# Six MoE chunks written out in a row in place of an engine loop with conditional arms

## Chip, cores and metric

The kernel runs on one core of one Trainium2 chip. The metric is the device time of one launch in microseconds (us), as the median of several runs.

## What is computed

Three stages follow each other. Sliding-window attention (4 batches, 8 heads, 576 positions, head size 64, window 64) gives x, one row of 512 for each of 2304 tokens. A dense gated layer maps it to new rows, and a mixture of 8 experts, one chosen per token, gives the output.

```
x = attention(q, k, v)                       # [2304, 512]
a = x @ w1 ; b = x @ w2                      # [2304, 1024]
x = (a * b @ w3) @ w_out                     # [2304, 512]
logits = x @ w_gate ; e = argmax(logits)     # 8 experts
h  = max(x @ w1[e], 0)
out = gate_w * sigmoid(x @ w_output_gate)[e] * (h @ w2[e])
```

## The kernel before

Every fp32 product is made of three TensorE matmuls (`product3`, L428 to L431): the high part of one factor by the high part of the other, and the two mixed products of a high and a low part. ScalarE (ACT) rounds a tile to its high part on the way out of PSUM, VectorE (DVE) subtracts to get the low part. TensorE (PE) is given its work by an order written out by hand, and the other engines follow by semaphores.

The program has these stages.

1. The fold: w3 and w_out are multiplied into one matrix W (`Wh`, `Wl`), together with the gate columns. Beside it runs the attention of batch 0.
2. The chunks. The 2304 rows of the dense layer are six chunks of 384 (`CH`). Two batches of 576 rows make one pass of three chunks (`NSUP` = 2 passes, `NCH` = 3 chunks in each). For each chunk `chunk` runs 8 hidden tiles of 24 matmuls (x by w1 and x by w2, `hidden_tile`), then 6 row tiles of 24 matmuls (a*b by W, `row_tile`), 14 steps in all. The first chunk of a pass, and the third chunk of the first pass, also carry the attention of one batch, one piece per step (`attend` before the step's own work: scores, L479; `attend_end` behind it: transposes, L489, and the product with v, L500). The second chunk of a pass and the last chunk of all carry none. The last chunk (`final`) also prepares the weights of expert 0 and, in `rank` (L557), begins the routing.
3. Routing: DVE computes each token's place in a list sorted by expert (L953 to L1034), with two small groups of matmuls (L560, L571, and L630 later).
4. The slot loop (`for_slots`, L299): one turn per 128 sorted tokens, with a gather of rows, two expert products (`hidden`, `project`) and a scatter. SyncE (SP) loads the weights of the next expert into `raw` (L413).

PE, ACT, DVE and GpSimd (POOL) each run the chunks through `for_chunks` (L238 to L245). In the kernel before, this is a loop of the engine itself: its body holds the code of chunk 0, of chunk 1, and two arms under a condition, one for the third chunk of the first pass, and one for the third chunk of the second pass (which is `final`). Four chunks of code therefore stand in each engine's program, and six are run. The number of the pass, `si`, is a register, so a chunk's waits compare a semaphore with a value that is computed from it.

At the start of each chunk PE waits for the last low part of the attention (`o_lo`), for the row tiles of the chunk before to be copied out of PSUM (`xB_ok`, `xA_ok`) and for the weights (`w12_lo`). The first chunk of a pass wants every ACT copy of the chunk before (`xA_ok` at `cc * CT + 1`), since its first hidden tile writes the banks that those copies read; the other chunks want all but the last two (L514). The copies are L730.

SP has its own loops for loading q, k, v and the expert weights.

Of the kernel before, what the change touches and what calls it, by code (L numbers as in the profile page):

```python
# [29 lines left out]
def build(nc, B, H, S, qT_in, kT_in, v_in, w1, w2, w3T_in, w_out, w_outT, w_gate, w_ogate, ew1, ew2, out):  # L30
# [13 lines left out]
    NSUP = N // SUPER  # L44
    CH = 384
    NCH = SUPER // CH
# [23 lines left out]
    with ctx:  # L70
# [164 lines left out]

        def for_chunks(eng, chunk):  # L238
            with eng.Fori(0, NSUP) as si:
                chunk(si * NCH, 0, si * 2 + 1, si * 2 + 1, 1, False)  # L240
                chunk(si * NCH + 1, 1, si * 2 + 2, None, 0, False)
                with eng.If(si < NSUP - 1):
                    chunk(si * NCH + 2, 2, si * 2 + 2, si * 2 + 2, 0, False)
                with eng.If(si > NSUP - 2):
                    chunk(si * NCH + 2, 2, si * 2 + 2, None, 0, True)  # L245


        def group_cols(k, parity):
# [69 lines left out]
        def _(sp):  # L318
# [5 lines left out]
            def load_w12(i):  # L324
                _, _, wr, src, kt = w12[i]
                if i >= KD:
                    sp.wait_ge(wo_lo, KF)
                sp.dma_start(wr[:, kt * FF:(kt + 1) * FF], src[kt * P:(kt + 1) * P, :]).then_inc(w12_in[i], 16)
# [96 lines left out]
        def _(pe):  # L425
# [131 lines left out]
            def rank():  # L557
# [2 lines left out]
                pe.matmul(bank[4][:, 0:TE], upper[:, :], oh[:, :], start=True, stop=True)  # L560
                pe.matmul(bank[5][:, 0:TE], ones[:, :], oh[:, :], start=True, stop=True).then_inc(rt_pe, 1)

            for_chunks(pe, chunk)

            pe.wait_ge(xA_ok, NT + 1)

# [73 lines left out]
        def _(act):  # L640
# [28 lines left out]
            def hi_w12(i):  # L669
                wh, wl, wr, _, kt = w12[i]  # L670
                ws = slice(kt * FF, (kt + 1) * FF)
                act.wait_ge(w12_in[i], 16)
                act.activation(wh[:, ws], wr[:, ws], ACT.Copy).then_inc(w12_hi, 1)
# [45 lines left out]
            def chunk(cc, c, batches, b, parity, final):  # L719
# [18 lines left out]
                for n, tt, i in row_tiles:  # L738
                    around(attend, attend_end, b, KF + i, parity, lambda: row_tile(i, n, tt))

            for_chunks(act, chunk)


            act.wait_ge(rt, 2)
# [62 lines left out]
        def _(dve):  # L807
# [36 lines left out]
            def lo_w12(i):  # L844
                wh, wl, wr, _, kt = w12[i]
                ws = slice(kt * FF, (kt + 1) * FF)
                dve.wait_ge(w12_hi, i + 1)
                dve.tensor_tensor(wl[:, ws], wr[:, ws], f32(wh[:, ws]), ALU.subtract).then_inc(w12_lo, 1)
# [56 lines left out]
            def chunk(cc, c, batches, b, parity, final):  # L905
# [22 lines left out]
                for n, tt, i in row_tiles:  # L928
                    around(attend, attend_end, b, KF + i, parity, lambda: row_tile(i, n, tt))

            for_chunks(dve, chunk)


            step = [0]
# [153 lines left out]
        def _(pool):  # L1088
# [49 lines left out]
            def attend(b, k, parity):  # L1138
                if k < NG:
                    pool.wait_ge(rec_ok, b * NG + (k + 1))  # L1140
                    pv = prob[k % 4][:, :].rearrange("p (i c) -> p i c", c=P)
                    pool.tensor_tensor(pv, pv, rec[:, k % 4 * 3:k % 4 * 3 + 3].unsqueeze(2).broadcast_to([P, 3, P]), ALU.mult).then_inc(p_ok, 1)  # L1142


            def split_lo(e, part):
                for c in range(NP1):
                    lo, hi = wcol(e, part, 1, c * PC), wcol(e, part, 0, c * PC)
                    pool.wait_ge(ew_hi[part], e * NP1 + c + 1)
                    pool.tensor_tensor(wbuf[:, lo:lo + PC], raw[part * NP1 + c][:, :], f32(wbuf[:, hi:hi + PC]),
                                       ALU.subtract).then_inc(ew_lo[part], 1)  # L1150
# [4 lines left out]
            def chunk(cc, c, batches, b, parity, final):  # L1155
                if b is not None:
                    for k in range(NG):
                        attend(b, k, parity)
                if final:
                    split_lo(0, 1)  # L1160
                for t in range(CT):
                    pool.wait_ge(xA_ok, cc * CT + (t + 2))
                    pool.wait_ge(xB_ok, cc * CT + (t + 2))
                    pool.dma_start(x_dram[bass.ds(cc * CH + t * P, P), :], x_sb[t][:, :]).then_inc(x_stored[t], 16)
                for t in range(CT):
                    pool.wait_ge(x_stored[t], cc * 16 + 16)
                pool.sem_inc(x_free, 1)

            for_chunks(pool, chunk)


            pool.wait_ge(idx_ok, 1)
# [82 lines left out]
```

## Time and profile before

| | |
|---|---|
| median of 3 runs | 778.92 us |
| the 3 runs | 777.67, 778.92, 780.96 us |
| span of the profiled execution, first to last instruction | 779.9 us |
| TensorE busy in the span | 731.2 us |
| mean granted TensorE clock | 0.970 |
| instructions in the profile | 15017 |

No time of the profiled execution other than its span is given; the span stands 1.0 us above the median of the runs. Times in a profile are from the start of the span. A busy time of PE counts overlapping matmuls once; a matmul starts before the end of the one ahead of it, so the distance between two starts is what one costs. "issue" as the releaser of an idle time says that the engine waited for nothing that the profile shows.

### The profile page before, as it was taken

Reading aid. Unit: us, or ns where it says so; the run is one execution under the profiler, and the core shown is the slowest. Engines: PE = TensorE matmul, PEld = TensorE weight load, DVE = VectorE, ACT = ScalarE, POOL = GpSimd, SP = SyncE. Lnnn points to the kernel's source line nnn. Section 1 sums busy time; section 2 is a strip of 40 time slices with the busy share of each in tenths; the row PEclk is TensorE's granted clock in tenths of the full one; section 3 lists DMA queues with packets and bytes.
Section 4 is the critical chain, followed back from the end, with each engine's and each line's share of the span. In section 5 each row is a group of like instructions: output and inputs, shape, how many; then the busy total and the mean of one; then the engine's idle time right before and its main releaser. Section 6 shows DMA issues by size and latency. Waiting matters only on the chain.

```text
span 779.9 us, 15017 instructions
## 1 busy us (share of the span) xinstructions
PE 731.2 (94%) x4832; PEld 670.9 (86%) x4833; DVE 333.0 (43%) x633; ACT 298.1 (38%) x720; POOL 141.3 (18%) x199
## 2 busy tenths in 40 slices
PE   6999999999999959999998975799999999999994
PEld 5999999999999959999998975688888888888883
DVE  3577444322154414541211279454456654562120
ACT  3577444422144414442201242044354554542221
POOL 7022011100111101111000054312221222121111
PEclk9999999999999979999999996699999999999998
DMA  9986222310112421206001052244446572611110
GB/s 292 234 245 168 57 61 77 95 41 1 42 32 58 114 76 32 58 28 224 34 7 38 0 194 104 94 149 151 147 136 217 200 234 88 219 32 40 30 41 27
DMA packets 64204, 80.27 MB, mean 103 GB/s; under 512 B 23501, under 2 KB 43981, under 8 KB 64144
## 3 DMA queue, kind: packets, MB, share of 16 engines
q1 hardware_dynamic: 59104, 64.01, 26.9%
q0 software_dynamic: 5040, 15.47, 5.9%
q8 instruction: 37, 0.61, 0.4%
q14 instruction: 23, 0.19, 0.1%
HBM read 70.03 MB, written 10.49 MB: 103 GB/s over the span
## 4 chain that ended last, share of the span: by engine, by line
PE 92%; DVE 4%; issue 2%; ACT 1%; DMA 0%; POOL 0%; DVEq 0%; POOLq 0%; ACTq 0%
PE bank L429 26%; PE bank L431 25%; PE bank L430 25%; PE bank L479 5%; PE bank L500 3%; PE bank L599 2%; PE bank L489 2%; DVE scll L1013 1%; PE bank L579 1%; PE bank L441 1%; PE bank L630 1%; PE bank L571 0%; DMA w3r<-in_w3T 0%; PE bank L467 0%; PE bank L463 0%
## 5 line engine op out<-in xcount | busy, mean ns | idle before, releaser
L429 PE MATMUL bank<-Wh,abh 128*128 128x272 f32 (+1 forms) x288 | 84.3, 293 | 0.0
L651 ACT ACTIVATE prob<-prob,nmx 128x128 f32<-128x128 f32 x144 | 56.3, 392 | 71.8 <-DVE nmx L821 71.8
L431 PE MATMUL bank<-Wh,abl 128*128 128x272 f32 (+1 forms) x288 | 82.4, 286 | 0.0
L430 PE MATMUL bank<-Wl,abh 128*128 128x272 f32 (+1 forms) x288 | 82.1, 285 | 0.0
L1142 POOL TENSOR_TENSOR prob<-prob,rec 128x384 f32<-128x384 f32 x48 | 39.8, 830 | 227.2 <-DVE rec L831 227.2
L429 PE MATMUL bank<-wbuf,xsTh 128*128 (+1 forms) x176 | 71.6, 407 | 0.7 <-DVE xsTl L1040 0.7
L1050 DVE TENSOR_TENSOR hTl<-bank,hTh 128x512 fp32r<-128x512 f32 x44 | 28.4, 686 | 101.2 <-ACT hTh L764 97.5
L902 DVE TENSOR_TENSOR wbuf<-raw,wbuf 128x1024 f32 (+1 forms) x56 | 66.0, 1222 | 12.8 <-ACT wbuf L716 12.8
L911 DVE TENSOR_TENSOR ab_f<-bank,a_sb 128x384 f32<-128x384 f32 x48 | 26.8, 558 | 104.2 <-PE bank L431 104.2
L429 PE MATMUL bank<-wbuf,hTh 128*128 x176 | 70.7, 402 | 0.0
L429 PE MATMUL bank<-xTh,w1h 128*128 128x384 f32 x192 | 67.8, 353 | 2.1 <-issue 2.0
L431 PE MATMUL bank<-wbuf,xsTl 128*128 (+1 forms) x176 | 69.7, 396 | 0.0
L430 PE MATMUL bank<-wbuf,xsTh 128*128 (+1 forms) x176 | 69.2, 393 | 0.0
L431 PE MATMUL bank<-wbuf,hTl 128*128 x176 | 68.9, 391 | 0.0
L430 PE MATMUL bank<-wbuf,hTh 128*128 x176 | 68.7, 390 | 0.0
L430 PE MATMUL bank<-xTl,w1h 128*128 128x384 f32 x192 | 65.5, 341 | 0.0
L431 PE MATMUL bank<-xTh,w1l 128*128 128x384 f32 x192 | 65.3, 340 | 0.0
L429 PE MATMUL bank<-xTh,w2h 128*128 128x384 f32 x192 | 64.3, 335 | 0.0
L430 PE MATMUL bank<-xTl,w2h 128*128 128x384 f32 x192 | 64.3, 335 | 0.0
L431 PE MATMUL bank<-xTh,w2l 128*128 128x384 f32 x192 | 64.2, 335 | 0.0
L716 ACT ACTIVATE wbuf<-raw 128x1024 f32 (+1 forms) x64 | 63.7, 1054 | 0.0
L724 ACT ACTIVATE abh<-ab_f 128x384 fp32r<-128x384 f32 x48 | 25.2, 525 | 90.1 <-DVE ab_f L911 90.1
(181 smaller groups left out, 1582.7 us busy)
## 6 DMA issues: line engine op xcount, KB each, us to landing
raw<-in_expert_w SPq DMA_DIRECT2D x64, 512.0 KB, 4.4
qbd<-in_qT SPq DMA_DIRECT2D x32, 144.0 KB, 3.7
kT<-in_kT SPq DMA_DIRECT2D x16, 288.0 KB, 4.1
x_rows<-x_sb POOLq DMA_DIRECT2D x18, 256.0 KB, 2.7
w3r<-in_w3T SPq DMA_DIRECT2D x8, 512.0 KB, 3.6
vA<-in_v SPq DMA_DIRECT2D x16, 256.0 KB, 3.0
vB<-in_v SPq DMA_DIRECT2D x16, 256.0 KB, 3.5
wo<-in_w_out SPq DMA_DIRECT2D x8, 256.0 KB, 6.9
```

The lines of the kernel that those rows point to most:

```text
L429: pe.matmul(dst, lh, rh, start=first, stop=False)
L430: pe.matmul(dst, lh, rl, start=False, stop=False)
L431: return pe.matmul(dst, ll, rh, start=False, stop=last)
L479: mm = pe.matmul(bank[4][:, (i % 3) * P:(i % 3 + 1) * P], qbd[r][:, i * P:(i + 1) * P], kT[r][:, key_start(i):key_start(i) + P], start=Tru ...
L500: mm = pe.matmul(bank[6 + k % 2][h * D:(h + 1) * D, i * WIN:(i + 1) * WIN], vt[:, h * D:(h + 1) * D], pT[(k - 1) % 2][:, i * P + h * WIN:i ...
L651: ex_i = act.activation(prob[k % 4][:, cols], prob[k % 4][:, cols], ACT.Exp, bias=nmx[:, row], accum_out=sums[:, row])
L716: act.activation(wbuf[:, bass.ds(wcol(e, part, 0, c * PC), PC)], raw[part * NP1 + c][:, :], ACT.Copy).then_inc(ew_hi[part], 1)
L724: act.activation(abh[:, f * CH:(f + 1) * CH], ab_f[f % 2][:, :], ACT.Copy).then_inc(ab_hi, 1)
L902: dve.tensor_tensor(wbuf[:, bass.ds(wcol(e, part, 1, c * PC), PC)], raw[part * NP1 + c][:, :], f32(wbuf[:, bass.ds(wcol(e, part, 0, c * PC ...
L911: dve.tensor_tensor(ab_f[f % 2][:, :], hidden_bank(c, f, 1)[:, 0:CH], a_sb[f % 2][:, :], ALU.mult).then_inc(ab_ok, 1)
L1050: dve.tensor_tensor(hTl[last][:, cols], bank[3 + n][:, :], f32(hTh[last][:, cols]), ALU.subtract).then_inc(hT_lo, 1)
L1142: pool.tensor_tensor(pv, pv, rec[:, k % 4 * 3:k % 4 * 3 + 3].unsqueeze(2).broadcast_to([P, 3, P]), ALU.mult).then_inc(p_ok, 1)
```

## The change

`for_chunks` no longer takes an engine and no longer opens a loop. It calls `chunk` six times in Python, with numbers in place of the register, so that each engine's program holds the six chunks one behind the other. The order of work is the same, and so are all waits; the values waited for are now constants. SP's loops and the slot loop stay as they are. The file is one line shorter, so that line numbers behind L245 are one less (L479 of before is L478 now).

```diff
-        def for_chunks(eng, chunk):
-            with eng.Fori(0, NSUP) as si:
-                chunk(si * NCH, 0, si * 2 + 1, si * 2 + 1, 1, False)
-                chunk(si * NCH + 1, 1, si * 2 + 2, None, 0, False)
-                with eng.If(si < NSUP - 1):
-                    chunk(si * NCH + 2, 2, si * 2 + 2, si * 2 + 2, 0, False)
-                with eng.If(si > NSUP - 2):
-                    chunk(si * NCH + 2, 2, si * 2 + 2, None, 0, True)
+        def for_chunks(chunk):
+            for cc in range(NSUP * NCH):
+                si, c = divmod(cc, NCH)
+                final = cc == NSUP * NCH - 1
+                batches = si * 2 + (1 if c == 0 else 2)
+                b = None if c == 1 or final else batches
+                chunk(cc, c, batches, b, 1 if c == 0 else 0, final)
...
-            for_chunks(pe, chunk)
+            for_chunks(chunk)
...
-            for_chunks(act, chunk)
+            for_chunks(chunk)
...
-            for_chunks(dve, chunk)
+            for_chunks(chunk)
...
-            for_chunks(pool, chunk)
+            for_chunks(chunk)
```

Two places of PE's program show what moves. The first is the end of a pass. (Names ending in h and l are high and low parts; `L239` is the loop, `L242` and `L244` are the two conditions.) Before, behind the code of chunk 2 (the first arm) PE leaves the arm and, in the first pass, jumps from the row `L244 COMPARE_AND_BRANCH` over the second arm, 351 rows of the program:

```order
L430 MATMUL bank<-Wl,abh 128x256
L431 MATMUL bank<-Wh,abl 128x256
L242 UNCONDITIONAL_BRANCH
L244 COMPARE_AND_BRANCH
L513 ISA [waits o_lo]
L514 REGISTER_ALU [waits xB_ok]
L429 MATMUL bank<-xTh,w1h 128x384 [waits W_lo,w12_lo,xA_ok]
```

It lands on the row `L239 REGISTER_ALU`, and the branch behind that takes it back to the loop's start, some 1615 rows up:

```order
L430 MATMUL bank<-Wl,abh 128x256
L431 MATMUL bank<-Wh,abl 128x256
L244 UNCONDITIONAL_BRANCH
L239 REGISTER_ALU
L239 COMPARE_AND_BRANCH
```

```order
L239 ISA
L513 ISA [waits o_lo]
L476 ISA [waits w12_lo,xA_ok,xB_ok]
L477 REGISTER_ALU [waits qk_in0]
L479 MATMUL bank<-kT_68,qbd_66 128x128 [waits masked]
```

Now, on PE, from the last row tile of chunk 2 to chunk 3:

```order
L428 MATMUL bank<-Wh,abh 128x256
L429 MATMUL bank<-Wl,abh 128x256
L430 MATMUL bank<-Wh,abl 128x256
L478 MATMUL bank<-kT_68,qbd_66 128x128 [waits w12_lo,qk_in0,xA_ok,masked,xB_ok,o_lo]
L478 MATMUL bank<-kT_68,qbd_66 128x128 x2
L428 MATMUL bank<-xTh,w1h 128x384 [waits W_lo]
```

The branches and register instructions are gone, and the scores of the next batch stand right behind the last matmul of chunk 2, with the same waits.

The second place is PE between chunk 4 and chunk 5. Before, the first condition is false in the second pass, so PE jumps from its row over the whole first arm, 457 rows, to the row `L244 COMPARE_AND_BRANCH` shown above and goes on into chunk 5 from there:

```order
L429 MATMUL bank<-Wh,abh 128x256
L430 MATMUL bank<-Wl,abh 128x256
L431 MATMUL bank<-Wh,abl 128x256
L242 COMPARE_AND_BRANCH
L513 ISA [waits o_lo]
L514 REGISTER_ALU [waits xB_ok]
```

Now the matmul that opens chunk 5 follows chunk 4 directly:

```order
L429 MATMUL bank<-Wl,abh 128x256
L430 MATMUL bank<-Wh,abl 128x256
L428 MATMUL bank<-xTh,w1h 128x384 [waits w12_lo,xA_ok,W_lo,xB_ok,o_lo]
L429 MATMUL bank<-xTl,w1h 128x384
L430 MATMUL bank<-xTh,w1l 128x384
```

PE's program grows from 2444 rows to 3120.

## Rows read from the trace of the kernel before

**Rows 1.** The page: PE's busy time, its clock by fortieths, the chain's shares.

```profile
PE 731.2 (94%) x4832; PEld 670.9 (86%) x4833; DVE 333.0 (43%) x633; ACT 298.1 (38%) x720; POOL 141.3 (18%) x199
...
PEclk9999999999999979999999996699999999999998
...
PE 92%; DVE 4%; issue 2%; ACT 1%; DMA 0%; POOL 0%; DVEq 0%; POOLq 0%; ACTq 0%
```

**Rows 2.** The waits: three of PE's (total us, times, longest).

```profile
PE bank L479 <- issue: 8.3, 1, 8.3
...
PE bank L560 <- DVE oh L961: 5.2, 1, 5.2
...
PE bank L429 <- issue: 2.0, 1, 2.0
```

**Rows 3.** The timeline, 275 to 290 us (start, duration, engine; idle before).

```profile
275.35 0.49 ACT L659 ACTIVATE pT<-bank 128x384 f32<-128x384 f32 x1
...
275.89 0.20 PEld L500 LDWEIGHTS bank<-pT,vB 128*64 128x64 f32 x4 [0.22 <-ACT pT L659]
...
279.21 0.28 PE L431 MATMUL bank<-Wh,abl 128*128 128x256 f32 x1
...
279.53 0.38 ACT L730 ACTIVATE x_sb<-bank 128x256 f32<-128x256 f32 x1 [2.69 <-PE bank L431]
...
287.84 1.64 PE L479 MATMUL bank<-kT,qbd 128*128 128x128 f32 x6 [8.35 <-issue]
...
289.60 0.52 PE L430 MATMUL bank<-xTl,w1h 128*128 128x384 f32 x1
```

**Rows 4.** The timeline of PE, 412 to 416 us.

```profile
412.19 0.28 PE L430 MATMUL bank<-Wl,abh 128*128 128x256 f32 x1
412.31 0.28 PE L431 MATMUL bank<-Wh,abl 128*128 128x256 f32 x1
...
414.57 0.41 PE L429 MATMUL bank<-xTh,w1h 128*128 128x384 f32 x1 [1.98 <-issue]
...
415.41 0.52 PE L430 MATMUL bank<-xTl,w1h 128*128 128x384 f32 x1
```

**Rows 5.** Windows cut from chunk starts to ACT copies: us, engines, PEclk, DMA, GB/s.

```profile
157.17:202.61 45.44, 45.44 (x293) 45.44 (x292) 10.45 (x22) 8.54 (x17) 0.54 (x1) 1.00 0.04 11
361.59:407.04 45.45, 45.45 (x293) 45.45 (x292) 10.45 (x22) 8.54 (x17) 0.54 (x1) 1.00 0.24 90
414.57:461.66 47.09, 46.97 (x288) 46.78 (x288) 17.18 (x29) 15.74 (x24) 6.02 (x3) 0.96 0.17 56
85.85:152.86 67.01, 67.01 (x541) 64.43 (x540) 31.13 (x81) 30.34 (x112) 10.74 (x13) 1.00 0.23 65
208.01:275.02 67.01, 67.01 (x541) 64.42 (x540) 30.79 (x80) 30.32 (x111) 11.08 (x14) 1.00 0.24 69
287.84:357.28 69.44, 69.33 (x539) 66.23 (x540) 30.78 (x80) 30.07 (x110) 10.54 (x13) 0.97 0.13 38
```

**Rows 6.** The DMA queues that bring instructions: 279.5 to 288, then 412.4 to 414.6.

```profile
q8 instruction: 3, 0.05, 3.5%
q14 instruction: 5, 0.04, 1.8%
...
q14 instruction: 1, 0.01, 1.5%
```

**Rows 7.** All DMA queues in 530 to 740 us, and the slot loop's scatters there.

```profile
q1 hardware_dynamic: 8320, 20.97, 30.5%
q0 software_dynamic: 2720, 7.88, 11.3%
...
out<-y_sb,sidc POOLq DMA_INDIRECT x17, 2.8
```

**Rows 8.** A short idle time of PE, and the window that holds it.

```profile
506.21 0.49 PE L429 MATMUL bank<-wbuf,xsTh 128*128 x1 [0.66 <-DVE xsTl L1040]
...
504.00:508.00 4.00, 3.34 (x21) 2.69 (x20) 1.66 (x4) 0.98 (x2) 1.21 (x2) 1.00 0.16 50
```

## The prediction

> **What bounds the kernel now.** I read the page first. TensorE is busy for 731.2 of 779.9 us and holds 92% of the chain that ended last [rows 1]. So the time is TensorE's, and a change counts only for what it takes out of, or puts into, TensorE's own row of work. The interesting part of the chain's shares is small: "issue" 2%, time in which an engine waited for nothing that the profile shows. The clock line has one dip between the start and the routing stage, a 7 in the fifteenth fortieth, which is 273 to 292 us.
>
> Next the list of waits, for PE alone. In the stretch of the chunks (86 to 475 us) it has two entries under "issue": 8.3 us once before the scores L479, and 2.0 us once before L429. The other long one there, 5.2 us before L560, is for DVE's routing work [rows 2]. The edit touches no operation of that work.
>
> Then the timeline at those two entries. The first is the end of the first pass: the last matmul of chunk 2 starts at 279.21 and the first scores of chunk 3 at 287.84 [rows 3]. The second lies between chunk 4 and chunk 5: 412.31 to 414.57 [rows 4]. Both are places where PE's program jumps, over an arm of 351 rows and back over 1615 rows at the first, over an arm of 457 rows at the second. Last I cut windows that hold equal work at each pass, and asked which DMA queues move in the gaps. The first shows what a gap costs behind it, the second what the engines are waiting for.
>
> **What the change removes.**
>
> *The jump back, directly.* PE cannot start chunk 3 right behind chunk 2, with or without the loop: its first hidden tile writes the banks that the last ACT copy reads, and it waits for that copy. The copy L730 runs from 279.53 to 279.91 [rows 3]. How long PE needs from ACT's end to its own start I take from the same rows: pT ends at 275.35 + 0.49 = 275.84 and L500 that waits for it starts at 275.89, so 0.05. Chunk 3 can start at 279.91 + 0.05 = 279.96. It starts at 287.84. Removed: **7.88 us**. All other conditions of that start are older: no wait but this one is listed there, and the profile calls the time issue. In the gap eight packets go over the instruction queues [rows 6]: the engines are fetching the code that they jumped to.
>
> *The jump back, behind it.* After the gap the clock is at its lower level (1.2 of 2.4 GHz): a matmul of 384 columns shows 0.52 us at 289.60. What that costs is read off equal work. From the first scores of a chunk with attention to its second L730, chunk 0 takes 67.01 us and chunk 2 67.01, both at clock 1.00; chunk 3 takes 69.44 at 0.97 [rows 5]. Removed, if TensorE does not idle long enough for the clock to fall: 69.44 - 67.01 = **2.43 us**. This holds a short second pause in it too.
>
> *The jump over the arm, directly.* Between chunk 4 and chunk 5 nothing has to be waited for (the copies that chunk 5 wants are two older ones). The distance between starts of row matmuls is 412.31 - 412.19 = 0.12, so chunk 5 could start at 412.43; it starts at 414.57 [rows 4]. Removed: **2.14 us**. One instruction packet falls into the gap [rows 6].
>
> *The jump over the arm, behind it.* The clock falls again (0.52 us for a matmul at 415.41, [rows 4]). From chunk start to first L730 chunk 1 takes 45.44 us and chunk 4 45.45, chunk 5 takes 47.09 at clock 0.96 [rows 5]. The last chunk is the one with `rank`, but that comes behind the fourth row tile, whose result this first L730 copies, so the TensorE work is equal. Removed: 47.09 - 45.45 = **1.64 us**.
>
> *Register work.* All engines lose the additions and register compares of the waits. On PE they cost nothing now: chunks 0, 1, 2 and 4 are busy for all of their windows (45.44 of 45.44, 67.01 of 67.01) [rows 5]. On ACT, DVE and POOL they stand in idle time, since these engines are busy for at most half of any such window. I set 0.
>
> **What it adds.** Two more chunks of code are fetched in place of being jumped back to. The first pass runs its code straight through and PE never idles in the windows of chunks 0 to 2 [rows 5], so fetching in a line is covered by the matmuls at hand. Chunk 4 is run straight through as well, while the expert weights come in (90 GB/s against 11 in chunk 1), and takes 45.45 against 45.44, so that load does not uncover it. If that cover failed once at a place, it would cost what the small gap costs, 2.14 + 1.64 = 3.8 us; not less than 0, since nothing here can speed a full row of matmuls up.
>
> What stays is the true wait at chunk 3: TensorE's last start 279.21 plus 0.12 to 279.96, some 0.6 us. Does it lower the clock? The nearest row is an idle time of 0.66 us at 505.5, and the window around it is at clock 1.00 [rows 8], while 1.98 us at 414.57 is followed by the lower level. I take no loss; the bound is one fall, 1.64 to 2.43 us.
>
> The chunk stage feeds later ones by semaphores alone. Routing and slot loop start from the end of the last chunk's tiles, and all of it moves forward as a block. The q, k and v loads of batch 3 are issued from the progress of batch 2 and have no row in PE's waits; they lose 8 us of slack at chunk 3, but at chunk 2, which starts with no gap in front of it, loads issued in the same rhythm leave PE busy for all 67.01 us. The eight loads of expert 0's weights follow the last attention tile, which also moves, and are wanted only at the end of the last chunk.
>
> **Sum.** 7.88 + 2.43 + 2.14 + 1.64 = 14.09 us. The span would go from 779.9 to 765.8; the median of the runs stands 1.0 below the span of before, so I predict 778.92 - 14.09 = **764.8 us**, 1.8% less.
>
> **The rivals.**
>
> 1. *One part of the gain is not got* (chance 0.12). Either the 0.6 us wait at chunk 3 does lower the clock, or one fetch in the straight code comes late, in one place where loads are heavy. Speaking for it: chunks 3 and 5 have never run directly behind their predecessors, and rows 8 is a single case, in the slot stage. Against: no idle time in the straight windows. Times: 764.8 + 2.4 = 767.2, or 764.8 + 3.8 = 768.6.
>
> 2. *The gaps are not due to the jumps* (0.03), but to some condition that the profile does not see at the start of chunks 3 and 5; then it stays and the time is 778.9. For it: "issue" is only what is left when no releaser is found. Against: the instruction packets in the gaps, the absence of any gap at chunks 1, 2 and 4, which check the same semaphores, and that the two gaps stand at the only long jumps. The Trainium skill (Advanced Engine Details and Errata, section Control Flow Timing) gives an unconditional branch about 51 ns and a compare with branch about 108 ns. By it alone the three branches of the first place and the one of the second would be worth an estimated 0.4 us, and the time would be 778.5. The trace shows gaps of 7.88 and 2.14 us, so a branch's own time is not what is paid there.
>
> 3. *The slot loop begins to fetch* (0.02), which makes it slower. The change moves the slot loop to another place in each engine's program. Today no instruction packet is seen in 210 us with 17 turns of it, only the two data queues are listed [rows 7], so each engine keeps the body at hand. If at the new place the body of one engine no longer fitted into what is kept, each turn would pay a fetch. At the price of the small jump, 2.14 us, 17 turns are 36 us, and the time 764.8 + 36 = 801. It decides from the seventh turn on (7 x 2.14 = 15). Against it: TensorE's body is 100 rows, against arms of 351 and 457 that are not kept. The Trainium skill (Runtime: NRT & Kernel Launch, section Instruction fetch mechanics) says that a taken branch stalls when its target is outside of a window of two pages of 256 instructions. By that rule the body of 100 rows, each matmul a load and a product, would still fit at any place, and nothing would be lost.
>
> 4. *More is gained* (0.03): DVE's routing chain shares its stretch with POOL's weight work, and a shift of one against the other may take a few us off; both follow the same tiles, so I expect no shift. About 761.
>
> **Numbers.** Forecast 0.80, rivals 0.12, 0.03, 0.02 and 0.03. The forecast's own spread is that of the runs, about 1.6 us each way, and 0.5 for the terms: 762.5 to 767. The range reaches over rival 1: **762 to 768.6**. A measurement of this kernel can tell about 0.5%, 3.9 us, from no change. Faster than 775.0: forecast, rivals 1 and 4, 0.95; within: rival 2, 0.03; slower: rival 3, 0.02.
>
> **What would show it.** Right: no "issue" wait before the scores or before L428 in PE's list; PE's distance from the last row matmul of chunk 2 to the scores about 0.7 us; chunk 3's window 67.0 us and chunk 5's 45.4 at clock 1.00; the dip of the clock line at the fifteenth fortieth gone; the routing and slot stages as long as before; PE busy time down by 4 us, the idle time by 10. Wrong: a gap of microseconds at either place with the branches gone (rival 2), instruction packets between 520 and 730 us and a turn of the slot loop longer than now (rival 3), or a clock below 1.00 behind the start of chunk 3 (rival 1).

## The result and the profile after

The changed kernel takes 766.92 us (median of 4 runs, 765.91 to 769.78), the kernel before 778.59 beside it: a ratio of 0.984, 95% interval 0.981 to 0.987, or 11.7 us. Two further comparisons on two other chips gave 767.51 against 779.04 (0.985, 0.983 to 0.987) and 767.01 against 779.78 (0.983, 0.981 to 0.985). All 14 times of the changed kernel have a median of 767.3, the 38 of the kernel before 779.4. The gain is thus about 12 us: 12.1 between these two medians, 11.5 to 12.8 chip by chip. 764.8 was forecast.

The page of the changed kernel, with the lines that answer to [rows 1]:

```profile
span 765.9 us, 14554 instructions
...
PE 727.4 (95%) x4832; PEld 667.9 (87%) x4833; DVE 332.5 (43%) x633; ACT 297.8 (39%) x720; POOL 139.5 (18%) x199
...
PEclk9999999999999999999999985799999999999998
...
PE 94%; DVE 3%; ACT 1%; DMA 0%; issue 0%; POOL 0%; POOLq 0%; DVEq 0%; ACTq 0%
```

The dip of the clock in the fifteenth fortieth is gone, "issue" has left the chain (2% to 0%), and TensorE does its 4832 matmuls in 3.8 us less of busy time, about what it had lost at the lower clock.

PE's waits, as in [rows 2]; times are total, count, longest:

```profile
PE bank L559 <- DVE oh L960: 5.2, 1, 5.2
...
PE bank L478 <- issue: 0.6, 1, 0.6
```

The idle time of 8.3 us before the scores is now 0.6, the 2.0 us before the first matmul of chunk 5 have no row any more, and the wait for the routing is as long as it was. The timeline at the start of chunk 3 (start, duration, engine; idle before), which answers to [rows 3]:

```profile
278.83 0.28 PE L430 MATMUL bank<-Wh,abl 128*128 128x256 f32 x1
...
279.14 0.38 ACT L729 ACTIVATE x_sb<-bank 128x256 f32<-128x256 f32 x1 [2.69 <-PE bank L430]
...
279.73 0.91 PE L478 MATMUL bank<-kT,qbd 128*128 128x128 f32 x6 [0.63 <-issue]
```

and at the start of chunk 5, which answers to [rows 4]:

```profile
401.83 0.28 PE L430 MATMUL bank<-Wh,abl 128*128 128x256 f32 x1
401.95 0.33 PE L428 MATMUL bank<-xTh,w1h 128*128 128x384 f32 x1
```

Last, windows cut as in [rows 5] (us; busy times and counts of PE, of its weight loads PEld, and of DVE, ACT, POOL; clock; DMA): chunk 2, chunk 3, and chunk 5.

```profile
207.62:274.64 67.02, 67.02 (x541) 64.44 (x540) 30.65 (x80) 30.35 (x112) 11.00 (x14) 1.00 0.24 68
...
279.73:346.80 67.07, 67.07 (x539) 64.49 (x540) 30.65 (x80) 29.96 (x110) 11.00 (x14) 1.00 0.16 45
...
401.95:447.32 45.37, 45.34 (x290) 45.14 (x288) 17.09 (x29) 16.12 (x25) 6.48 (x4) 1.00 0.16 56
```

Chunk 3 now takes what chunk 2 takes, and both are at full clock. Between 520 and 730 us only the two data queues move, as in [rows 7]:

```profile
q1 hardware_dynamic: 8320, 20.97, 29.5%
q0 software_dynamic: 2739, 7.89, 11.5%
```

### The profile page after: what moved, and what is told of

Read it like the earlier page. It is cut to its first block, busy times and chain, and to the rows that moved or that the text cites. A ratio compares the mean times of both kernels' runs of the same rounds, so it can differ in the third digit from the quotient of the medians.

```text
span 765.9 us, 14554 instructions
## 1 busy us (share of the span) xinstructions
PE 727.4 (95%) x4832; PEld 667.9 (87%) x4833; DVE 332.5 (43%) x633; ACT 297.8 (39%) x720; POOL 139.5 (18%) x199
## 4 chain that ended last, share of the span: by engine, by line
PE 94%; DVE 3%; ACT 1%; DMA 0%; issue 0%; POOL 0%; POOLq 0%; DVEq 0%; ACTq 0%
PE bank L428 26%; PE bank L430 26%; PE bank L429 26%; PE bank L478 5%; PE bank L499 3%; PE bank L598 2%; PE bank L488 2%; DVE scll L1012 1%; PE bank L578 1%; PE bank L440 1%; PE bank L629 1%; PE bank L570 0%; DMA w3r<-in_w3T 0%; PE bank L466 0%; PE bank L462 0%
## 5 line engine op out<-in xcount | busy, mean ns | idle before, releaser
L429 PE MATMUL bank<-Wl,abh 128*128 128x272 f32 (+1 forms) x288 | 82.3, 286 | 0.0
```

The lines of the kernel that those rows point to most:

```text
L429: pe.matmul(dst, lh, rl, start=False, stop=False)
```

## The experiments

My theory was that TensorE waits for the code that it jumps to, and that the lower clock behind each gap follows from the idle time. The rivals were another engine's jump, the register work of the waits, and a condition that the profile does not see.

**Whose jump it is.** In e1 only TensorE's chunks are written out (`straight_chunks` are the changed kernel's six calls); e2 is the mirror.

```diff
-            for_chunks(pe, chunk)
+            straight_chunks(chunk)
```

> Only TensorE's six chunks are written out; ACT, DVE and POOL keep the loop. If TensorE's own jump makes the gaps (my theory): TensorE starts chunk 3 within 1 us of the last row matmul of chunk 2; the others pay their fetch beside two hidden tiles (10 us) that need nothing of them but the masked scores, so at most 2 us of new waits near the second step of chunk 3: 767 to 770 us. If the gaps come from the other engines' jumps, or from a condition that they set: 778 us, and the gap stands.

Measured: 767.05 us (766.64 to 767.90), ratio 0.985 (0.982 to 0.988), beside 767.51 for the full change on the same chip. The timeline of e1 shows TensorE start chunk 3 with no more delay than in the changed kernel, while DVE, which still jumps, takes the scores up at 281.80, 2.1 us behind their start, where it is 0.95 us in the changed kernel (280.68 behind 279.73):

```profile
279.68 0.57 PE L488 MATMUL bank<-kT,qbd 128*128 128x128 f32 x3 [0.63 <-issue]
...
281.80 0.56 DVE L827 SCALAR_TENSOR_TENSOR prob<-bank,mask 128x384 f32<-128x384 f32 x1 [5.01 <-issue]
```

DVE's delay is covered: TensorE has its own hidden tile to do. The whole gain is had from one engine. The page's counts of instruction packets say which queue is whose. Queue q8 has 37 packets in the kernel before and 30 in e1 and in the changed kernel, so it brings TensorE's code. Queue q14 has 23 in the kernel before and in e1, and 13 in the changed kernel, so it brings that of the other engines.

> The mirror of the run with only TensorE written out: TensorE keeps the loop, ACT, DVE and POOL have six chunks in a row. If TensorE's own jump makes the gaps: both gaps stand, 7 to 8 us and 2 us, and the time is that of before, 778 us (a little less if the engines' fetches hinder each other). If the other engines' jumps make them: 767 us.

Measured: 780.37 us (778.61 to 781.53), ratio 1.000 (0.999 to 1.002). Both gaps stand in PE's waits:

```profile
PE bank L488 <- issue: 7.9, 1, 7.9
...
PE bank L438 <- issue: 2.0, 1, 2.0
```

So writing out the other three engines is worth nothing here, and their fetches do not lengthen TensorE's idle time by more than it varies anyway (7.9 to 8.5 us over five traces, below).

**Whether it is the registers.** e3 keeps six chunks in a row, with waits of PE, ACT and DVE computed from a register that is always 0 plus a number. (Where DVE writes the logits, the column is a constant.)

```diff
+            z = eng.snap(eng.to_reg(0), min_val=0, max_val=NSUP - 1)
+            for n in range(NSUP * NCH):
+                si, c = divmod(n, NCH)
+                s = z + si
...
+                chunk(s * NCH + c, c, batches, b, 1 if c == 0 else 0, final)
```

> Six chunks in a row as in the changed kernel, but PE, ACT and DVE compute what they wait for from a register, as the loop did (about 100 register instructions on each; POOL has constants). If register work is free beside the matmuls: 766.9 us, no difference to the changed kernel. If part of the gain came from the constants: up to 100 x 0.05 = 5 us slower on TensorE, 772, spread over all steps.

Measured: 767.22 us (766.57 to 768.33), ratio 0.985 (0.983 to 0.988), beside 767.51 for the changed kernel on the same chip. Register work is free beside these matmuls.

**Whether a jump alone makes a gap.** e5 is the changed kernel with three jumps of TensorE over code that never runs, at places that had none and where nothing is waited for.

```diff
+                    rows = {1: 24, 2: 160, 4: 456}.get(cc)
+                    if rows:
+                        with pe.If(z > 0):
+                            for _ in range(rows):
+                                pe.matmul(bank[7][:, 0:P], abh[:, 0:P], abl[:, 0:P], start=True, stop=True)
```

> The changed kernel, in which TensorE jumps over code that is never run: 24 products before chunk 1, 160 before chunk 2, 456 before chunk 4 (each a load and a product, under a register that is always 0). At these three places no jump stood before and no wait holds TensorE. Theory (a jump pays for code that is not at hand): nothing at 24, up to 2.1 us at 160, about 2.1 us and the lower clock behind it (1.6) at 456; 770 to 775 us. Rival (the gaps belong to chunks 3 and 5, by a condition unseen): no gap at any of the three, 767.

Measured: 773.71 us (772.17 to 774.77), ratio 0.992 (0.990 to 0.994), some 6.4 us more than the changed kernel's 767.3 on other chips. The timeline before chunk 1 (24 products skipped) and before chunk 2 (160) has no gap, that before chunk 4 (456) has one of 4.1 us:

```profile
156.89 0.28 PE L430 MATMUL bank<-Wh,abl 128*128 128x256 f32 x1
157.01 0.33 PE L428 MATMUL bank<-xTh,w1h 128*128 128x384 f32 x1
...
207.73 0.28 PE L430 MATMUL bank<-Wh,abl 128*128 128x256 f32 x1
207.85 0.83 PE L478 MATMUL bank<-kT,qbd 128*128 128x128 f32 x6
...
351.23 0.28 PE L430 MATMUL bank<-Wh,abl 128*128 128x256 f32 x1
355.62 0.66 PE L428 MATMUL bank<-xTh,w1h 128*128 128x384 f32 x1 [4.11 <-issue]
```

The two near branches cost TensorE nothing that is seen; the far one does. This refutes the rival "the gaps belong to chunks 3 and 5": chunk 4 never had a gap before. Behind the gap the clock is down. The window from there to the first ACT copy is 47.95 us at 0.94, where chunk 4 of before has 45.45 at 1.00 [rows 5]:

```profile
355.62:403.57 47.95, 47.95 (x290) 47.95 (x291) 10.45 (x22) 8.15 (x17) 0.00 (x0) 0.94 0.15 56
```

So this one jump costs 4.27 + 2.50 = 6.77 us in the trace, against 6.4 in the times (4.27 is the distance of 4.39 us between the two starts, less 0.12). The time came out in the range expected, but the price is more than the 2.1 + 1.6 = 3.7 us that were expected. One thing differs at this place: expert weights are loaded at full rate, and their queue holds the DMA engines for 93.5% of the time between 351.4 and 355.7. Whether that lengthens the gap was not tried.

**One long jump in place of two.** e4 takes the last chunk out of the loop, so the first pass ends in a single jump back.

```diff
-                with eng.If(si > NSUP - 2):
-                    chunk(si * NCH + 2, 2, si * 2 + 2, None, 0, True)
+            chunk(NSUP * NCH - 1, 2, NSUP * 2, None, 0, True)
```

> On all engines the last chunk stands behind the loop, so that the first pass ends with one long jump (back) where the kernel before has two (over the last chunk's arm, then back). If each long jump pays its own fetch: the gap at chunk 3 shrinks by the price of the small one, from 7.9 to 5.7 us, the gap before chunk 5 stays at 2.1, and the time is 776.5 us. If one fetch sets the whole gap: 7.9 stays and the time is 778.6.

Measured: 776.01 us (774.33 to 776.98), ratio 0.995 (0.994 to 0.997). The time came out as written, the gap did not: it fell from 7.9 or more to 3.4 us, not to 5.7.

```profile
PE bank L478 <- issue: 3.4, 1, 3.4
...
PE bank L428 <- issue: 1.9, 1, 1.9
```

So each jump pays. By subtraction, of the 8 us in the kernel before the jump over the last chunk's arm made some 4.5 and the jump back 3.4, the true wait of 0.6 us included; this takes it that the two add up and that the jump back costs the same when the last arm no longer lies in the loop. In the traces the third copy of chunk 3 comes 76.8 us behind that of chunk 2 (279.7 to 356.5), against 82.3 before, 5.5 us less, while the medians differ by 4.0: here too the trace of before shows a larger cost than the medians do (see below).

**Fetching ahead.** e7 is e4 with an instruction at the top of each pass that names where the loop's branch goes.

```diff
-            with eng.Fori(0, NSUP) as si:
+            with nc.Fori(0, NSUP, engines=[eng.engine], hint_back_edge=True) as si:
```

> The kernel with the last chunk behind the loop, plus one instruction at the top of each pass on every engine that names the place the loop's branch will go to, so that its code can be fetched ahead. It changes nothing but where code is fetched. Theory: most of the gap at chunk 3 goes (under 1.5 us in place of some 5.7) and the clock behind it stays up; the small gap before chunk 5 stays; about 770 us. Rival (the gap is the branch itself or a condition): no change to the kernel without the hint, 776 us.

Measured: 771.10 us (770.59 to 772.02), ratio 0.990 (0.987 to 0.992), 4.9 us less than e4 on the same chip. The timeline at chunk 3:

```profile
280.46 0.93 PE L478 MATMUL bank<-kT,qbd 128*128 128x128 f32 x6 [0.72 <-issue]
...
282.65 0.33 PE L430 MATMUL bank<-xTh,w1l 128*128 128x384 f32 x1 [0.92 <-issue]
```

The jump back goes to the same place as in e4, and 3.4 us of idle time became 0.72 (most of it the true wait) and 0.92 two matmuls later. Naming the target ahead changes no wait and no work, so the idle time belongs to getting at the code behind the jump, not to a wait or to the branch. In what way the hint helps is not shown: TensorE's queue q8 has 35 packets in both kernels, while q14, that of the other engines, goes from 18 to 13.

Not all of the 4.9 us are the hint's at this jump. From the last copy of chunk 2 to that of chunk 3 e7's trace is 3.4 us shorter than e4's (73.4 against 76.8). The other 1.6 us lie behind the gap before chunk 5. That gap stays, as expected, with 1.8 us, but this time the clock does not fall behind it, and the window of chunk 5 is 45.46 us at 1.00, where e4 has 47.01 at 0.96:

```profile
PE bank L428 <- issue: 1.8, 1, 1.8
...
405.76:451.22 45.46, 45.42 (x288) 45.23 (x288) 17.09 (x29) 15.73 (x24) 5.94 (x3) 1.00 0.18 58
```

Nothing in the edit accounts for that part. In b3, a trace of the kernel before, the gap there is also 1.8 us long and the clock does fall (47.14 us at 0.96).

**The wait that stays.** e6 is the changed kernel with banks chosen by `cc` in place of `c`, so that chunk 3 need not wait for the last copy.

```diff
-                pe.wait_ge(xA_ok, cc * CT + (1 if c == 0 else 1 - 2))
+                pe.wait_ge(xA_ok, cc * CT + (1 if cc == 0 else 1 - 2))
...
-            return bank[(2 * (c + f) + m) % 4]
+            return bank[(2 * (cc + f) + m) % 4]
```

> The changed kernel with PSUM banks turned by the number of the chunk, not by its place in the pass, so that chunk 3 no longer writes the banks that the last copies of chunk 2 read, and need not wait for them. Theory: the idle time of 0.63 us before chunk 3's scores goes, the rest stays: 0.7 us faster than the changed kernel, about 766.2. Rival: the start of chunk 3 is then bound by another wait or by the fetch of code, and nothing changes.

Measured: 767.06 us (765.49 to 767.12), ratio 0.984 (0.982 to 0.986), beside 767.51 and 0.985. In the trace the wait is gone:

```profile
278.77 0.28 PE L430 MATMUL bank<-Wh,abl 128*128 128x256 f32 x1
278.89 0.83 PE L478 MATMUL bank<-kT,qbd 128*128 128x128 f32 x6
```

The scores follow at 0.12 us in place of 0.90, 0.8 us earlier. The times (0.45 us apart on the same chip) agree in sign with that and with the 0.7 us expected, but are too close to tell it from nothing. It is the version to keep: no slower, and one wait less.

**The size of the gain.** The changed kernel again, and on a third chip with three more profiles of the kernel before.

> The changed kernel itself, timed again beside the kernel before on one chip, to size the gain. From the two traces (start of chunk 3 earlier by 8.1 us, its window shorter by 2.4, start of chunk 5 earlier by a further 2.1, and 1.6 behind it, less 0.4 that is lost again at the routing): 14 us, a ratio of 0.982. The first three rounds gave 11.7 us between the medians; if the smaller number is the true one, something outside of the span (before the first or behind the last instruction) takes 2 us back, and the clocked time stands further above the span than in the kernel before.

> The kernel before itself, for another profile. The two traces shown differ by 14.0 us of span, the medians of all runs by 11.5 to 11.7, and the clocked time stands 1.7 us above the span in both kernels, so the profiled execution of before was some 2 us longer than its median. Theory A: the length of the two gaps varies from execution to execution, since fetches from memory do, and the first trace caught long ones; then the gap here is up to 2 us shorter than 8.35, with the same stages around it. Theory B: the gaps are the same within 0.3 us and the stages before the chunks or behind them vary.

> As b1_before, a second execution: the gap before the scores of chunk 3, the gap before chunk 5, and the stages around them. Theory A: they differ from one another by up to 2 us. Theory B: within 0.3 us.

> As b1_before, a third execution. With four traces of the kernel before, the mean cost of the two jumps can be set against the measured gain of 11.6 us: Theory A expects 11 to 12.5 us, Theory B 14.

> The changed kernel on the same chip as the three profiles of before, for the same comparison: chunk 3's first scores 0.9 us behind the last row matmul, equal windows, and a ratio of 0.985 (11.6 us), as on the two chips so far. Were the true gain 14 us, the ratio would be 0.982.

Measured: a0 767.51 us (0.985) and a1 767.01 us (0.983), both given above. The idea in a0's expectation that something outside of the span takes 2 us back does not hold: the clocked time stands 1.6 to 1.9 us above the span in all runs of both kernels. The three profiles of before have spans of 779.3, 780.3 and 779.5 us. The longest waits of PE under "issue", in b1, b2 and b3:

```profile
PE bank L479 <- issue: 8.1, 1, 8.1
```

```profile
PE bank L479 <- issue: 8.5, 1, 8.5
```

```profile
PE bank L479 <- issue: 7.9, 1, 7.9
```

The gap before chunk 5 was 1.8 to 2.0 us. From the last ACT copy of chunk 2 to that of chunk 3 the four traces of before take 82.3, 82.0, 82.8 and 82.2 us and three of the changed kernel 72.2 each time; from the last copy of chunk 4 to the first of chunk 5 it is 49.0, 49.1, 49.0 and 48.9 against 45.2 three times. The gain within the chunks is therefore 10.15 + 3.8 = 14.0 us in the mean, with 0.8 between the traces. That is neither theory's number in full: the gaps vary by 0.6 us, more than B wanted and less than A. The stages before the first copy vary by 0.4 us between the four traces of before, those from the first copy of chunk 5 to the end by 0.5; in the changed kernel's three by 0.9 and 1.0.

## Why the prediction was right

**What bounds the kernel** held: no work was taken away, and the time fell by what TensorE no longer idled or ran slowly.

**The jump back, directly** (7.88 us). From the last row matmul to the scores it was 8.63 us and is 0.90, so 7.73 went. The start came 0.15 us later than I worked out from the copy's end and 0.05 for the semaphore.

**Behind it** (2.43 us): the window went from 69.44 to 67.07, 2.37 us.

**The jump over the arm** (2.14 and 1.64 us): from 2.26 us between two starts to 0.12, 2.14 us; the window from 47.09 to 45.37, 1.72 us.

The four sum to 13.96 us by the two traces, where I had 14.09; 14.0 is the difference of the spans. Each term was read where the time was. e1, e2 and e5 show that TensorE's own far jumps are the cause, and e7 that their idle time is that of getting at the code behind them.

**Register work at 0** held (e3). **The code that is added at 0** held: no "issue" in the windows of chunks 3 and 5. **The true wait at chunk 3 does not lower the clock** held (1.00). The rivals 2 and 3 are out: no gap without a jump, and no instruction packet in the slot loop. By its time alone 766.92 would fit rival 1 too (767.2), but neither of its two causes is there: chunk 3 runs at 1.00, and TensorE is busy for 67.07 of 67.07 us in its window and for 45.34 of 45.37 in that of chunk 5. Nor was 761 seen, the time of rival 4.

The Trainium skill (Advanced Engine Details and Errata, section Control Flow Timing) gives a branch some 51 or 108 ns. At the two near jumps of e5 the trace does not show even that: the matmuls stay 0.12 us apart. The far jumps of these runs cost 1.8 to 4.5 us each.

**What was misread** is the one instruction packet in the gap before chunk 5 [rows 6]. It is on q14, and that is not TensorE's queue (e1). TensorE's own packet comes just ahead of the gap, between 411.3 and 412.7 us:

```profile
q8 instruction: 1, 0.02, 5.8%
```

From 412.7 us until TensorE starts at 414.57 its queue brings nothing. In e2 no instruction packet of any engine falls between 412.0 us and the start at 413.87, and the gap stands there with 2.0 us. The long gap is alike: three of its eight packets are TensorE's, and from 285.1 us to 287.8, just before the start, no DMA queue moves anything at all:

```profile
DMA packets 0, 0.00 MB, mean 0 GB/s; under 512 B 0, under 2 KB 0, under 8 KB 0
```

So the transfer of code fills only a part of a gap. What passes in its last 1.9 and 2.8 us is not shown by any run. The terms of the sum do not depend on it, since they were read from the whole gaps.

**What was off** is the step from the trace to the median. I wrote that the median stands 1.0 us below the span. In fact the clocked time stands some 1.7 us above its own span in both kernels (1.6 to 1.9; 779.89 with 778.3, 767.51 with 765.7), so the traced execution of before, whose own time is not given, was by this estimate one of some 781.6 us, 2.7 above the median. A sum that is true of it, 14 us, was then taken off the median, and the medians differ by 12.1; these 2 us are what lies between 764.8 and 766.92. The three other traces of before were long ones too (781.0 to 781.9 beside a median of 779.8 on that chip), and the changed kernel's trace there was 1.0 above its median. On that chip the traces give 779.7 - 766.3 = 13.4 and the medians 12.8; on the other two chips the medians give 11.7 and 11.5. Whether an execution that is 2 us shorter has shorter gaps, or shorter stages elsewhere, stays open. None of the five traces with both jumps is of a short execution; the nearest to its median is that of e2 (780.9 beside 780.4), and its gap of 7.9 us is at the short end (its way from the last copy of chunk 2 to that of chunk 3 is 81.7 us, the shortest of the five), but b3, a long one, shows 7.9 as well.

Nothing of note was given back later. From the start of chunk 5's first ACT copy to the end of its last, the kernel before takes 13.31 us at clock 0.87, and the changed kernel 13.70 at 0.75:

```profile
447.32:461.02 13.70, 8.16 (x52) 7.98 (x52) 11.99 (x28) 1.15 (x4) 5.18 (x4) 0.75 0.55 184
```

But the matmuls L571 (L570 now), which the routing goes on with, start 13.66 us behind that first copy before and 13.75 now, so that 0.1 us is left of the 0.4. In the other traces it is 13.6 to 13.7 us before, and 13.65 and 14.43 in the changed kernel. The expectation for a0 counted the 0.4 us as lost.

## What to carry to other kernels

A long idle time under "issue" on the bounding engine, at a loop's end or at a skipped arm, is a sign that it waits for the code behind a far jump. Here it cost its own length and then, where the clock fell, 1.6 to 2.5 us more. Only the engine that bounds had to be written out straight: the others' delays were hidden, since it had work of its own behind the jump. Where the code cannot grow, move one-off arms behind the loop and name the branch's target with a hint. Together these got 9 of the 12 us here, of which, in the trace, 1.6 came because the clock did not fall behind the gap that stayed.

## What the runs showed of the hardware

- The price of a far jump on TensorE was not one number: 1.8 to 2.1 us over an arm at one place (the skipped arm is that of chunk 2, 588 matmuls), 4.1 us over one of 456 matmuls at another, 3.4 us for the jump back alone, 7.9 to 8.5 for two in a row (the last two with a true wait of 0.6 us in them). So a longer skip was not the dearer one. What sets the price within that range was not tried.
- A jump over 160 products (320 instructions, each product a load and a matmul) cost nothing, one over 456 at another place did. No length in between was tried.
- The instruction packets fill only a part of these gaps: between TensorE's last one and its next matmul lay 1.9 us in the short gap of the kernel before and 2.8 us in the long one.
- After the gaps of 1.9 us and more TensorE ran at the lower of its two levels (1.2 GHz) for 3.4 to 5.4 us, longest in e5. After idle times of 0.63 to 0.92 us it did not. A gap of 1.8 us was followed by the lower level in b3 and not in e7.
- A profiled execution can stand up to 2.2 us above the median of its kernel (b2: 781.93 beside 779.78), and by the estimate above 2.7. An absolute forecast should be built from the clocked time that belongs to the trace.
